# Attention and two MLPs in float32 on one core: first weight halves later, the small constant summed in as a pair, new orders at the attention's end and in the second quad

## The reference

```python
q_d, k_d, v_d = (t.reshape(B, H, S // 4, 4, D).mean(axis=3) for t in (q, k, v))
out_d = sm_attn(q_d, k_d, v_d)            # a = exp(s - max); a / (sum(a) + 1e-09)
mask = np.abs(pos[:, None] - pos[None, :]) < 4
attn = exp(where(mask, scores, -1e9) - max)
attn = attn / (np.sum(attn, axis=-1, keepdims=True) + 1e-09)
x = np.repeat(out_d, 4, axis=2) + attn @ v
h = x @ w_in;  x = (h - np.tanh(h)) @ w_out                       # 512 -> 2048 -> 512
gate = 1.0 / (1.0 + np.exp(-(x @ w_gate)))
return (gate * (x @ w_val)) @ w_out2                              # 512 -> 1536 -> 512
```

## Time and profile before

| | us |
|---|---|
| median of 3 runs | 940.01 |
| the profiled execution, its own time | 939.61 |
| its span in the profile | 937.8 |
| PE, DVE, ACT, POOL busy | 898.9, 594.8, 386.9, 291.7 |

### The profile page before, as it was taken

One profiled execution on the slowest core, in us unless ns is written; L12 is line 12 of the kernel. 1 busy time (PEld: TensorE's weight loads), 2 busy tenths in 40 slices (PEclk: granted clock), 3 DMA queues, 4 the chain that ended last, 5 costly groups with the idle time before them and its releaser, 6 DMA issues.

```text
span 937.8 us, 15651 instructions
## 1 busy us (share of the span) xinstructions
PE 898.9 (96%) x6056; PEld 843.5 (90%) x6056; DVE 594.8 (63%) x918; ACT 386.9 (41%) x752; POOL 291.7 (31%) x237
## 2 busy tenths in 40 slices
PE   7879789999999999999998999999999999999997
PEld 5657679999999999999997999999999999999996
DVE  8779966767865657765668556566544456544444
ACT  4667664535432325332343544454222234222221
POOL 5687866683103000120016555732200001000000
PEclk9889888999999999999999999999999999999999
DMA  9867638568554546464421767779775555565511
GB/s 248 220 157 230 182 113 327 210 262 303 211 207 164 211 160 210 160 214 158 168 91 45 284 262 278 281 287 362 284 282 211 213 210 210 198 274 202 202 45 68
DMA packets 46089, 197.01 MB, mean 210 GB/s; under 512 B 3936, under 2 KB 15552, under 8 KB 33216
## 3 DMA queue, kind: packets, MB, share of 16 engines
q1 hardware_dynamic: 41984, 166.66, 49.4%
q0 software_dynamic: 4032, 29.36, 8.3%
HBM read 139.90 MB, written 56.10 MB: 209 GB/s over the span
## 4 chain that ended last, share of the span: by engine, by line
PE 84%; DVE 6%; POOL 4%; issue 3%; ACT 2%; DVEq 0%; ACTq 0%; POOLq 0%
PE banks L826 45%; PE banks L896 19%; PE banks L1012 16%; PE banks L804 1%; PE banks L781 1%; POOL prob L587 1%; DVE row_den L1342 1%; DVE qk_down L1327 1%; DVE row_max L1308 1%; PE banks L759 1%; DVE x_op L1360 1%; DVE row_sum L1334 1%; POOL v_four L580 1%; PE banks L817 1%; POOL prob_d L587 0%
## 5 line engine op out<-in xcount | busy, mean ns | idle before, releaser
L826 PE MATMUL banks<-x_op,pair 128*128 128x384 f32 x1512 | 278.5, 336 | 1.7 <-DVE cg_sum L1529 1.7
L826 PEld LDWEIGHTS banks<-x_op,pair 128*128 128x128 f32 x1512 | 266.7, 189 | 9.7 <-DVE cg_sum L1529 2.1
L896 PE MATMUL banks<-g_parts,mid 128*128 128x384 f32 x1152 | 227.8, 336 | 5.3 <-DVE x_all L1442 5.2
L896 PEld LDWEIGHTS banks<-g_parts,mid 128*128 128x128 f32 x1152 | 203.4, 189 | 7.1 <-DVE x_all L1442 7.1
L826 PE MATMUL banks<-x_op,win 128*128 128x384 f32 x1008 | 205.3, 340 | 2.7 <-ACT c_sum L1120 2.7
L826 PEld LDWEIGHTS banks<-x_op,win 128*128 128x128 f32 x1008 | 180.6, 192 | 3.6 <-ACT c_sum L1120 3.1
L1012 PE MATMUL banks<-wout,p_parts 128*128 128x512 f32 x648 | 163.6, 393 | 1.7 <-issue 1.7
L1442 DVE TENSOR_TENSOR x_all<-banks,x_all 128x384 f32<-128x384 f32 x168 | 92.8, 555 | 77.3 <-PE banks L896 76.7
L1012 PEld LDWEIGHTS banks<-wout,p_parts 128*128 128x128 f32 x648 | 120.2, 188 | 22.6 <-issue 2.1
L1554 DVE TENSOR_TENSOR x_all<-banks,x_all 128x512 f32<-128x512 f32 x90 | 62.1, 690 | 113.7 <-PE banks L1012 113.7
L1134 ACT ACTIVATE banks<-c_sum 128x384 f32<-128x384 f32 x72 | 35.2, 490 | 94.9 <-DVE c_sum L1409 49.2
(11 more groups left out here) (96 smaller groups left out, 1016.2 us busy)
## 6 DMA issues: line engine op xcount, KB each, us to landing
pair<-kept_pair SPq DMA_DIRECT2D x24, 1792.0 KB, 10.9
win<-kept_in SPq DMA_DIRECT2D x16, 1792.0 KB, 7.4
kept_pair<-pair SPq DMA_DIRECT2D x12, 1792.0 KB, 11.8
mid<-kept_mid POOLq DMA_DIRECT2D x16, 1024.0 KB, 5.1
kept_in<-win SPq DMA_DIRECT2D x7, 1792.0 KB, 5.8
wout<-kept_out POOLq DMA_DIRECT2D x12, 1024.0 KB, 11.8
kept_mid<-mid SPq DMA_DIRECT2D x7, 1024.0 KB, 6.8
kept_out<-wout SPq DMA_DIRECT2D x6, 1024.0 KB, 14.5
```

Of the source, the lines that this page charges most:

```text
L826: mm = pe.matmul(bk[:, 0:T], weights[:, w, p - 1, kk, :], x_op[:, p - 1, x, kk, :], start=(first and kk == 0 and a == 0), stop=(last and k ...
L896: mm = pe.matmul(bk[:, 0:T], w[:, wp, f, m * P:(m + 1) * P], g[:, gp, 2 * f + t, :], start=(f == 0 and a == 0), stop=(f == 1 and a == 2))
```

## The change

Five things are changed. (1) ScalarE's roundings of the first two weight tiles stand one to three turns later, and GpSimd's sums and lows of these tiles and SP's stores are moved to fit. (2) `row_sum` gets a second column that holds 1e-9, and `row_den` is the sum over each pair, where it was a scalar addition. (3) The highs of x for products 1, 7 and 6 stand in turns 12, 13 and 14 in place of 13, 13 and 16, and their lows in turns 13, 14 and 15. (4) TensorE makes product (0,1) in turn 15, between the transposes of unit 14, and ScalarE and VectorE have new orders in the last two turns. (5) ScalarE rounds weight tile 2 and plain tile 1 behind the copies of the second quad, where these roundings stood ahead of the first quad's tanh. The quads from n = 2 on keep their order.

```diff
-        row_sum = low.tile("row_sum", [P, COLS])
+        row_sum = low.tile("row_sum", [P, COLS, 2])
...
-                dve.tensor_scalar(row_den[:, :], row_sum[:, :], EPS, None, ALU.add).then_inc(s_den, 1)
+                dve.tensor_reduce(row_den[:, :], row_sum[:, :, :], AX_X, ALU.add).then_inc(s_den, 1)
...
+            dve.memset(row_sum[:, :, 1], EPS).then_inc(s_cols, 1)
...
# GpSimd
-                if 5 <= t < 9:
-                    first_weight_low(t - 5)
-                if t == 6:
+                if t == 5:
                     weight_sums(1, (0, 1))
-                if t == 7:
-                    weight_sums(1, (2, 3))
-                if t == 9:
+                if 6 <= t < 10:
+                    first_weight_low(t - 6)
+                if 7 <= t < 9:
+                    weight_sums(1, (t - 5,))
+                if t == 10:
                     plain_low(0)
...
-            weight_sums(2)
+            weight_sums(2, (0, 1))
             x_last_sum(0)
+            weight_sums(2, (2, 3))
# ScalarE
-                if 3 <= t < 5:
-                    half_weight_high(0, t - 3)
-                if 7 <= t < 9:
-                    half_weight_high(1, t - 7)
-                if t == 6:
+                if 4 <= t < 6:
+                    half_weight_high(0, t - 4)
+                if 10 <= t < 12:
+                    half_weight_high(1, t - 10)
+                if t == 7:
                     plain_high(0)
...
# VectorE, last turns and first quad
-                if t == 13:
-                    x_low(0, 1)
-                    x_low(0, 7)
+                if 13 <= t < 15:
+                    x_low(0, (1, 7)[t - 13])
...
+            second_weight_low()
+            x_low(0, 4)
+            add_c(0, C11)
+            add_c(0, C22)
+            g_tile(0, C11)
...
+            write_x(UNITS - 1)
# SP
-                if 8 <= u < 12:
+                if 10 <= u < 14:
...
-                if 12 <= u < 14:
-                    keep_early(kept_mid[0], flat_f32(mid[0][:, :, :, :]), s_mlo, 1, 2 * (u - 12))
+                if 11 <= u < 15:
+                    keep_early(kept_mid[0], flat_f32(mid[0][:, :, :, :]), s_mlo, 1, u - 11)
```

More of the change, by code:

```diff
@@ L522, in _ @@
                     load_raw(1)
[L523 to L527 removed]
+                if 10 <= u < 14:
+                    keep_early(kept_in[0], flat_f32(win[0][:, :, :, :, :]), s_wlo, lows(0), u - 10)
+                if 11 <= u < 15:
+                    keep_early(kept_mid[0], flat_f32(mid[0][:, :, :, :]), s_mlo, 1, u - 11)
                 if u == 14:
@@ L857, in first_product @@
                 elif p == 7:
+                    if n == 0:
+                        pe.wait_ge(s_exd, 4 * UNITS)
                     mm = product(c, w, p, True, False)
@@ L934, in _ @@
                     down_scores(t + 1)
+                if t == UNITS - 1:
+                    first_product(0, 1)
                 if t == UNITS:
@@ L1143, in g_high, with first_quad @@
                 act.activation(g_parts[n % 2][:, 0, pick, :], c_sum[n % 2][:, pick, :], ACT.Copy).then_inc(s_ghi, 1)
-            def first_quad(n, skip=0):
+            def first_quad(n):
                 last, s = n % Q1 == Q1 - 1, n // Q1 + 1
-                first = n % Q1 == 0 and n > 0
+                first = n % Q1 == 0
                 if n > 1:
                     g_high(n - 1, 1)
-                if skip < 1:
                     copy_c(n, C11)
-                if n == 1:
-                    g_high(0, 1)
                 if last:
@@ L1158, in first_quad @@
                     x_high(s - 1, 4)
-                if skip < 2:
+                if n > 1:
                     copy_c(n, C22)
@@ L1164, in first_quad @@
                     x_high(s - 1, 3)
-                if skip < 3:
+                if n > 1:
                     copy_c(n, C21)
@@ L1179, in first_quad @@
                 tanh(n, C12)
-                if 1 <= n and n + 1 < Q1:
+                if n + 1 < Q1:
                     plain_high(n + 1)
@@ L1189, in _ @@
                     copy_rest(t - 2, 1)
+                if t == UNITS:
+                    copy_c(0, C11)
+                    x_high(0, 2)
+                    x_high(0, 5)
                 if t == UNITS + 1:
                     x_high(0, 4)
+                    tanh(0, C11)
                 if t < UNITS:
@@ L1224, in _ @@
                     copy_c(0, C21)
-            first_quad(0, skip=3)
+            tanh(0, C22)
+            tanh(0, C21)
+            g_high(0, 0)
+            tanh(0, C12)
+            copy_c(1, C11)
+            g_high(0, 1)
+            copy_c(1, C22)
+            copy_c(1, C21)
+            act.wait_ge(s_vd, UNITS)
+            weight_high(2)
+            plain_high(1)
             for n in range(1, N1):
@@ L1366, in _ @@
                 dve.memset(prob[i][:, PROBS:PROBS + 4], 0.0).then_inc(s_cols, 1)
-            dve.memset(row_sum[:, :], 1.0).then_inc(s_cols, 1)
+            dve.memset(row_sum[:, :, 0], 1.0).then_inc(s_cols, 1)
+            dve.memset(row_sum[:, :, 1], EPS).then_inc(s_cols, 1)
             dve.wait_ge(s_band, 2)
@@ L1392, in _ @@
                 if t == UNITS:
-                    x_low(0, 6)
+                    x_low(0, 2)
+                    x_low(0, 5)
                 if t >= 2:
                     write_x(t - 2)
-            x_low(0, 2)
-            x_low(0, 5)
+                if t == UNITS - 1:
+                    x_low(0, 6)
             x_low(0, 3)
-            x_low(0, 4)
             def add_c(n, i):
@@ L1487, in first_quad @@
                     x_low(s, 2)
-            for n in range(N1):
+            second_weight_low()
[3 more added lines that the diff above has]
+            g_tile(0, C11)
+            add_c(0, C21)
+            g_tile(0, C22)
+            g_tile(0, C21)
+            g_low(0, 0)
+            g_tile(0, C12)
+            write_x(UNITS - 1)
+            for n in range(1, N1):
                 first_quad(n)
```

24 lines of the change are left out of this document (5 added, 19 removed).

## The result

The changed kernel takes 935.52 us (median of 20 runs, 929.12 to 941.40), the kernel before in the same comparison 941.81 us (20 runs, 937.34 to 946.98). The ratio is 0.9926, 95% interval 0.9904 to 0.9948: 6 to 7 us faster, where 16 were forecast, and outside the range of 914 to 932. The forecast of 924 started from three runs of the kernel before at 940.01; its 20 runs here have a median 1.8 us higher, so the time misses by 11.5 us, but the gain only by 9.7. The profiled execution of the changed kernel took 930.66 us (span 928.8), the third lowest of the 20.

A forecast was written before the change was run, and what follows sets the result against it. TensorE, busy 96% of the span, was taken as the bound, so the second quad's start decides: 22.7 us earlier less 6.5 given back makes 16.2 us. Forecast 924 us, range 914 to 932.

The forecast's parts named there:

- Term 4: Second quad: the moved roundings are late, TensorE pauses 6.5 us before block 4, then half clock; 6.5 us given back.
- term 1: Attention: weight halves later, ScalarE's two waits go, GpSimd leads; last scaling at 104.2, not 119.43, 15.2 us earlier.
- rival (c): Attention held by loads or the round trip, not GpSimd's work: turns 0.6 us longer, 6 us, 930; chance 0.17.
- term 3: Attention's end: 13.3 us from last scaling to the product in quad 1, at 117.5, not 140.16, 22.7 us earlier.
- Rival (b): Second quad gives nothing back, as tile 3's sums end before ScalarE needs them: 914.5; chance 0.13.
- (d): Pair sum waits for GpSimd like the scalar addition; GpSimd pauses 0.39 after nine turns, 3.5 us: 927.5; chance 0.07.
- (e): Second quad's lateness returns in each next quad, with pause and clock drop of 9.5 us: slower, 943; chance 0.03.

The follow-up runs named there:

- the quiet GpSimd: Changed kernel with GpSimd's sums of weight tile 2 held until all seven lows of x are made, and product 4's low ahead of the second weight low: 932.34 us, 0.9912.
- the one profile with 0.63: Changed kernel loading only one row of each v window from unit 2 on, so its output is another: 927.40 us, 0.9848.

## Why the prediction was wrong

**Right.** GpSimd leads from turn 6 on; undisturbed, turn 6 to the last scaling takes 62.1 us, and my sum had 61.5. The pair sum takes 0.17 us (0.2). ScalarE waits for no weight sum in turns 3 to 11. Term 4 held almost exactly: from product (1,6) to block 4 17.1 us (16.9), a pause of 6.51 (6.5), and 10.7 in place of 8.3 for the eight groups behind it, 2.4 (3.0). A little luck is in it: the steps that I wrote down add to 16.6 (13.1 + 3.5), and the low of plain tile 1 took 3.12 us where I had 2.35. Of the Trainium skill's rule, "SBUF — State Buffer", on SBUF's two separate sides, that one of the two waits for the whole instruction of the other, I weighed only GpSimd's side, where the rows again show 0.7 per low. On VectorE's side they show up to 3.0: a low of 0.94 us took 3.97.

**Wrong: term 1, "with 0.4 for one wait in turn 5", and 1 us for the load of tile 1 ("half a turn, the most that I allow for" was 3).** I placed the scaling of turn 6 at 42.7 (30.8, two turns of 4.56, 0.4, 1.4 and 1). Ten profiles with the same early program and all bytes have it at 44.6 to 52.4, mean 47.0; from there to the last scaling they take 62.0 to 66.2, mean 63.5. So the last scaling lies at 110.5 on average, 6.3 us behind the 104.2 predicted, 4.3 of them ahead of turn 6; the changed kernel's first profile, 107.75, was a lucky one. What stood there instead of 1.4 us: GpSimd waits 2.3 to 6.1 us for tile 1 in eight of the ten profiles, and TensorE up to 2.6 us for its instructions in seven, in several with the half clock behind it. The rows were there. In short stretches of the kernel before the DMA share (the last number but one) reads

```profile
12.00:24.00 12.00, 10.56 (x180) 0.86 0.98 235
24.00:36.00 12.00, 8.20 (x152) 0.90 0.99 237
```

and I took its mean over 123 us, 0.75, and concluded that transfers don't stop the kernel. This is my rival (c), given 0.17, with another mechanism: not q and v in turns 10 to 13, but tile 1 and TensorE's instructions in turns 4 to 8, made dearer by the clock.

**Wrong: term 3, "What remains behind the last scaling is the path of one unit".** 13.3 us to product (1,6) were 18.0 in the first profile and 16.5 in the second; the six profiles with this end have 17.3 on average, 4.0 more than the sum. I had counted TensorE's products and the unit's round trip, and left out VectorE's four lows and the weight low: 5.20 + 0.94 + 2.55 + 0.94 us nearly in a row, two of them beside GpSimd. The four profiles with the quiet GpSimd have 14.6 on average, which shows 2.7 of the 4.0 us; the other 1.3 go, by their rows, to the lows that still wait for GpSimd.

**The sum.** 6.3 and 4.0 put product (1,6) 10.3 us late; the median misses by 11.5, of which 1.8 are the three low runs that the forecast started from. What lies behind (1,6) was some 1 us shorter than worked out. The parts are means over profiles that spread by several us, so they agree with the whole to 1 or 2 us and no better. Rival (b) was refuted by the pause; (d) by the 168 ns; (e) did not come: behind block (1,0) the kernels are alike, though part 5 by itself costs 4.7 to 5.7 us. My terms held that: 6.5 us given back against the pause of 2.74 that it removes. I put both into one sum and did not see that this part alone loses.

## What to carry to other kernels

Read the DMA share in short stretches, not as a mean: where it is near 1, each wait for a load varies from execution to execution, and in one execution TensorE's half clock behind it made 3.8 us of lateness at turn 6 into 7.1 at the last scaling. Profile the same kernel twice before you explain a difference of a few us between two profiles. When a pause is moved, set its new price beside the old one, with everything queued behind it; a rounding that waits for another engine belongs behind the work that doesn't need it, and the loads that it needs ahead of the stores. And count every engine's own list of work behind the last late result, not only the bound engine's.

## What the runs showed of the hardware

- A VectorE subtraction with two SBUF inputs that takes 0.94 us alone took 3.97 beside GpSimd in the changed kernel. It waited from 110.95 to about 114.0 while three GpSimd additions ran one after another; VectorE did not get in between them. GpSimd's next addition then took 1.44 us in place of 0.72.
- An addition of a constant to 14 elements took 0.76 us on the median and up to 2.05 beside GpSimd, a reduction of 28 elements 0.17 in all 16 turns.
- TensorE stalled 0.7 to 3.3 us in the middle of a group without a wait, 15 times in 17 profiles, and each stall ended 1.36 to 1.75 us behind a 16 KB packet of an "instruction" queue. The DMA share ahead of these packets was 0.92 to 1.05; in the one profile with 0.63 no stall came.
